# Seeding matmul banks with partial sums, and moving product 4, in a mixture kernel of seven-product quads

## The reference

```python
x = attention(q, k, v, n_global, n_local)      # banded, with 8 global keys
x = x.transpose(0, 2, 1, 3).reshape(1536, 512)
h = x @ w_in                                   # 512 -> 2048
x = (h / (1 + np.exp(-h))) @ w_out             # 2048 -> 512
P = np.exp(x @ w_gate - max)                   # 1536 x 8
for _ in range(8):
    P /= P.sum(1, keepdims=True) + 1e-09
    P /= P.sum(0, keepdims=True) + 1e-09
    P *= N / E
for e in range(8):
    out += P[:, e:e+1] * (np.maximum(x @ w1[e], 0.0) @ w2[e])   # 512 -> 1024 -> 512
```

## Time and profile before

| | us |
|---|---|
| median of 3 runs | 1489.78 (1489.61 to 1491.42) |
| profiled execution | 1489.47 |
| its span, first to last instruction | 1487.7 |
| TensorE busy | 1395.9 |
| VectorE busy | 951.6 |
| ScalarE busy | 584.2 |
| GpSimd busy | 338.2 |

### The profile page before, as it was taken

How to read it: one execution, slowest core, us unless ns; L and a number is a source line. 1 busy time by engine, 2 the same in 40 slices (tenths; PEclk the granted TensorE clock), 3 DMA queues, 4 the chain that set the end, 5 groups by cost and what they waited for, 6 DMA issues and landing times.

```text
span 1487.7 us, 20276 instructions
## 1 busy us (share of the span) xinstructions
PE 1395.9 (94%) x7339; PEld 1272.7 (86%) x7339; DVE 951.6 (64%) x1562; ACT 584.2 (39%) x1148; POOL 338.2 (23%) x377
## 2 busy tenths in 40 slices
PE   6995899999998999999999999999999999999999
PEld 5885898989997889898888989888898988889897
DVE  6455948674938584664838567783856748385662
ACT  5564727363614142332414334351433415243331
POOL 4002413130403030412214031321403123140300
PEclk9998999999989999999999999999999999999999
DMA  8310222221211121212212121231212122221201
GB/s 188 83 43 1 78 64 64 64 78 57 65 36 43 50 90 60 71 57 64 65 51 92 57 72 57 69 102 57 85 57 72 57 64 65 64 79 57 74 26 50
DMA packets 63246, 97.81 MB, mean 66 GB/s; under 512 B 18608, under 2 KB 30896, under 8 KB 63152
## 3 DMA queue, kind: packets, MB, share of 16 engines
q1 hardware_dynamic: 63152, 96.57, 21.7%
HBM read 93.41 MB, written 3.15 MB: 65 GB/s over the span
## 4 chain that ended last, share of the span: by engine, by line
PE 59%; DVE 25%; issue 3%; ACT 3%; DVEq 0%; ACTq 0%
PE a_ps L915 12%; PE c_ps L915 11%; DVE parts L1107 8%; DVE up_l L1070 8%; PE d_ps L915 6%; PE b_ps L915 6%; PE d_ps L827 5%; DVE hid_l L1114 5%; PE a_ps L827 4%; PE c_ps L827 4%; PE a_ps L912 2%; PE d_ps L912 2%; PE c_ps L912 2%; PE b_ps L827 2%; DVE down_l L1075 1%
## 5 line engine op out<-in xcount | busy, mean ns | idle before, releaser
L811 POOL TENSOR_TENSOR up_sum<-up_sum 128x256 f32<-128x256 f32 x80 | 63.1, 789 | 943.7 <-DMA up_sum<-w_up 932.0
L1075 DVE TENSOR_TENSOR down_l<-down_raw,down_h 128x512 fp32r<-128x512 f32 x160 | 112.1, 711 | 205.6 <-ACT down_h L974 205.6
L1070 DVE TENSOR_TENSOR up_l<-up_sum,up_h 128x1024 fp32r<-128x1024 f32 (+1 forms) x160 | 217.3, 1368 | 3.6 <-ACT up_h L965 3.3
L974 ACT CAST down_h<-down_raw 128x512 fp32r<-128x512 f32 x160 | 95.4, 622 | 271.4 <-PE c_ps L915 230.9
L965 ACT CAST up_h<-up_sum 128x1024 fp32r<-128x1024 f32 (+1 forms) x160 | 149.0, 943 | 40.7 <-PE d_ps L827 31.6
L827 PE MATMUL d_ps<-xc_h,up_h 128*128 128x384 f32 x320 | 112.4, 351 | 53.6 <-DVE parts L1107 53.4
L1114 DVE SCALAR_TENSOR_TENSOR hid_l<-parts,hid_h 128x384 fp32r<-128x384 f32 x192 | 144.8, 780 | 8.0
L996 ACT COPY parts<-a_ps 128x384 f32<-128x384 f32 x80 | 37.3, 466 | 256.8 <-PE a_ps L827 256.8
L1002 ACT ACTIVATE hid_h<-parts 128x384 fp32r<-128x384 f32 x192 | 94.4, 520 | 106.7 <-DVE parts L1107 106.5
L827 PE MATMUL a_ps<-xc_h,up_h 128*128 128x384 f32 x320 | 109.9, 343 | 15.9 <-DVE xc_l L1102 14.7
L827 PEld LDWEIGHTS d_ps<-xc_h,up_h 128*128 128x128 f32 x320 | 60.4, 189 | 67.6 <-DVE parts L1107 65.0
(11 more groups left out here) (187 smaller groups left out, 3441.7 us busy)
## 6 DMA issues: line engine op xcount, KB each, us to landing
up_sum<-w_up SPq DMA_DIRECT2D x80, 512.0 KB, 3.5
down_raw<-w_down SPq DMA_DIRECT2D x160, 256.0 KB, 2.6
q_sb<-qT SPq DMA_DIRECT2D x12, 256.0 KB, 3.5
k_sb<-kT SPq DMA_DIRECT2D x24, 128.0 KB, 3.6
v_sb<-v SPq DMA_DIRECT2D x24, 128.0 KB, 3.5
out<-acc SPq DMA_DIRECT2D x12, 256.0 KB, 2.1
vg_sb<-v SPq DMA_DIRECT2D x16, 4.0 KB, 1.6
nraw<-n_global SPq DMA_DIRECT2D x1, 1.0 KB, 2.5
```

What stands on the lines that cost most here:

```text
L811: nc.gpsimd.tensor_tensor(w[2], w[3], w[6], ALU.subtract).then_inc(up_summed, 1)
L974: nc.scalar.copy(down_h[:, tile % DOWN_BUFS, :], down_raw[:, tile % DOWN_RAWS, :]).then_inc(down_h_ready, 1)
L1070: nc.vector.tensor_tensor(up_l[:, quad % 2, lo:hi, :, :], up_sum[:, quad % 2, lo:hi, :, :], up_h[:, quad % 2, lo:hi, :, :].bitcast(F32), A ...
L1075: nc.vector.tensor_tensor(down_l[:, tile % DOWN_BUFS, :], down_raw[:, tile % DOWN_RAWS, :], down_h[:, tile % DOWN_BUFS, :].bitcast(F32), A ...
```

## The change

- *Seeds.* ScalarE copies P1 from a_ps into b_ps, and P6 and then P7 are added on top of it by TensorE, so that b_ps holds U2 and then U3. ScalarE copies U2 to parts and U3 into d_ps, and P4 is added on top of that. VectorE keeps two sums per quad, C12 and C22. Three fp32 matmuls (`open_banks`) write the three banks once at the start.
- *Product 4* of a quad runs after P1 and P5 of the next quad; that of the last quad after three outputs of the first down tile. P1 and P5 of the next step's first quad run among the outputs of the last down tile. The order is P1, P5, P4 of the quad before, P6, P2, P3, P7.
- *Weights.* Three quads of split up weights are held instead of two. The weights of the next step's first three quads are summed and split in the down part, those of the fourth in the third quad (in step 0 those of the second and third in the quad before). There are three pieces (3, 2 and 2 slots) instead of two. Down weights have two buffers of raw tiles and four of split ones.
- *Sums.* VectorE makes the sums of the weights, GpSimd those of the first two quads and the first sums of x, during the attention of the second batch.
- *SiLU steps.* The rounded part of a hidden result is made by VectorE (`tensor_copy`) instead of ScalarE.
- The output's accumulator is kept in x_sb.

The diff, cut to its core. Of functions that were rewritten only the new lines stand here.

```diff
--- before.py
+++ after.py
@@ -18,8 +18,9 @@
 I32 = mybir.dt.int32
 SLOTS = 7
-DOWN_RAWS = 4
-DOWN_BUFS = 3
+RAWS = 2
+UP_BUFS = 3
+DOWN_BUFS = 4
 FAR = 1.0e30
...
+                    def sum_up(quad):
+                        w = [up_slot(quad, n) for n in range(SLOTS)]
+                        pool.wait_ge(up_in[quad], 16)
+                        then(nc.gpsimd.tensor_tensor(w[4], w[3], w[2], ALU.add))
+                        nc.gpsimd.tensor_tensor(w[6], w[0], w[3], ALU.subtract)
+                        then(nc.gpsimd.tensor_tensor(w[5], w[4], w[0], ALU.subtract))
+                        then(nc.gpsimd.tensor_tensor(w[3], w[1], w[5], ALU.subtract))
...
+                    gather_gaps(0)
+                    for qb in range(2, QB):
+                        pack(0, qb)
+                    gather_gaps(1)
+                    for quad in range(RAWS):
+                        sum_up(quad)
+                    for qb in range(2, QB):
+                        pack(1, qb)
+                        if qb == 2:
+                            pool.wait_ge(x_ready, QB + 1)
+                        sum_x(qb - 2)
...
+            RECIPE = {"P1": (0, 0), "P5": (4, 1), "P6": (5, 2), "P2": (1, 3), "P3": (3, 4), "P7": (6, 5), "P4": (2, 6)}
+            X_SUM_SLOT = {0: 1, 1: 2, 2: 5, 3: 6}
+            X_RAW_SLOT = {0: (0, 0), 3: (1, 0), 4: (1, 1)}
+            PIECES = ((0, 3), (3, 5), (5, 7))
...
+                    def open_banks():
+                        for ps in (b_ps[0], b_ps[1], d_ps):
+                            mm = nc.tensor.matmul(ps[:, 0:HALF], ident[:], x_sb[:, 0, 0:HALF], start=True, stop=True)
+                        mm.then_inc(opened, 1)
...
+                    def multiply(quad, name, ps, add):
+                        w, x = RECIPE[name]
+                        s = quad // FP
+                        pe.wait_ge(up_ready, len(PIECES) * quad + PIECE_OF[w] + 1)
+                        if quad % FP == 0 and s in turns:
+                            pe.wait_ge(xc_ready, SLOTS * turns.index(s) + x + 1)
                         n = 0
                         for k in range(2):
                             for a, b in ((up_h, xc_h), (up_h, xc_l), (up_l, xc_h)):
+                                mm = nc.tensor.matmul(ps[:, 0:HALF], a[:, quad % UP_BUFS, w, k, :], b[:, x, k, :],
                                                       start=(n == 0 and not add), stop=(n == 5), skip_group_check=True)
                                 n += 1
                         mm.then_inc(product, 1)
...
+                    def p4(quad):
+                        pe.wait_ge(kept, 4 * quad + 4)
+                        multiply(quad, "P4", d_ps, True)
+                    def others(s, i, after):
+                        quad, side = s * FP + i, i % 2
+                        pe.wait_ge(kept, 4 * quad + 1)
+                        multiply(quad, "P6", b_ps[side], True)
+                        multiply(quad, "P2", a_ps[side], True)
+                        if "P2" in after:
+                            after["P2"]()
+                        pe.wait_ge(kept, 4 * quad + 2)
+                        multiply(quad, "P3", c_ps[side], True)
+                        pe.wait_ge(kept, 4 * quad + 3)
+                        multiply(quad, "P7", b_ps[side], True)
...
+                                    if t == 3:
+                                        p4(quad3)
                                     pe.wait_ge(*bank_free[t])
                                 for n, (a, b) in enumerate(((0, 0), (0, 1), (1, 0))):
                                     start, stop = j == 0 and n == 0, j == FT - 1 and n == 2
@@ -916,6 +945,10 @@
                                                               start=start, stop=stop)
                                 if j == FT - 1:
                                     mm.then_inc(down_done, 1)
+                                    if s + 1 < STEPS and t == len(banks) - 3:
+                                        p1(s + 1, 0)
+                                    if s + 1 < STEPS and t == len(banks) - 2:
+                                        p5(s + 1, 0)
                                 elif t == len(banks) - 1:
...
+                    def keep_p1(s, i):
+                        quad = s * FP + i
+                        act.wait_ge(product, made[quad, "P1"])
+                        if s == 0 and i == 0:
+                            act.wait_ge(opened, 1)
+                        if i >= 2:
+                            act.wait_ge(summed, 2 * (quad - 2) + 2)
+                        elif s > 0:
+                            act.wait_ge(acc_ready, outs_before[s - 1] + 3 * i + 3)
+                        nc.scalar.copy(b_ps[i % 2][:, 0:HALF], a_ps[i % 2][:, 0:HALF]).then_inc(kept, 1)
...
+                    def keep_u3(s, i):
+                        quad = s * FP + i
+                        act.wait_ge(product, made[quad, "P7"])
+                        if i > 0:
+                            act.wait_ge(hid_ready, 4 * (quad - 1) + 4)
+                        elif s > 0 and outs[s - 1] == 8:
+                            act.wait_ge(acc_ready, outs_before[s - 1] + 8)
+                        elif s > 0:
+                            act.wait_ge(hid_ready, 4 * (quad - 1) + 4)
+                        nc.scalar.copy(d_ps[:, 0:HALF], b_ps[i % 2][:, 0:HALF]).then_inc(kept, 1)
...
+                    def hidden(s, i, n, src, value, f, half):
+                        quad = s * FP + i
                         if blocks[s][1] >= HALVES:
+                            nc.scalar.activation(hid_h[:, f, half, :], src, ACT.Relu).then_inc(hid_h_ready, 1)
                         else:
+                            if quad > 0 and n in (0, 3):
+                                act.wait_ge(hid_ready, 4 * (quad - 1) + n + 1)
+                            if i == 0 and s in turns and n == 0:
+                                act.wait_ge(xc_ready, SLOTS * turns.index(s) + X_SUM_SLOT[2] + 1)
                             nc.scalar.activation(value, src, ACT.Silu).then_inc(silu_ready, 1)
...
                     def quad_work(s, i):
                         quad = s * FP + i
+                        start = s == 0 and i == 0
+                        keep_p1(s, i)
+                        if start:
+                            split_x(0, 4)
+                        if i > 0:
+                            hidden22(s, i - 1)
+                        keep_p5(s, i)
+                        if start:
+                            split_x(0, 5)
+                            split_x(0, 6)
+                        if i > 0:
+                            hidden21(s, i - 1)
+                        if i == 2:
+                            split_up(quad + 1, 0)
+                        elif i < 2:
+                            split_down(s * FT + 2 * i)
+                        keep_u2(s, i)
                         if s == GATE and i == 1:
                             exp_gate()
+                        hidden11(s, i)
+                        if i == 2:
+                            split_up(quad + 1, 1)
+                        elif i < 2:
+                            split_down(s * FT + 2 * i + 1)
+                        if s == 0 and i < 2:
+                            for piece in range(len(PIECES)):
+                                split_up(quad + 1, piece)
+                        hidden12(s, i)
+                        keep_u3(s, i)
+                        if i == 2:
+                            split_up(quad + 1, 2)
...
+                    def sum_up(quad):
+                        if quad >= QUADS:
+                            return
+                        w = [up_slot(quad, n) for n in range(SLOTS)]
+                        before = 4 * (quad - RAWS)
+                        dve.wait_ge(up_in[quad % RAWS], 16 * (quad // RAWS) + 16)
+                        nc.vector.tensor_tensor(w[4], w[3], w[2], ALU.add).then_inc(up_summed, 1)
+                        nc.vector.tensor_tensor(w[6], w[0], w[3], ALU.subtract).then_inc(up_summed, 1)
+                        dve.wait_ge(up_summed, before + 1)
+                        nc.vector.tensor_tensor(w[5], w[4], w[0], ALU.subtract).then_inc(up_summed, 1)
+                        dve.wait_ge(up_summed, before + 3)
+                        nc.vector.tensor_tensor(w[3], w[1], w[5], ALU.subtract).then_inc(up_summed, 1)
...
+                    def add12(s, i):
                         quad = s * FP + i
+                        dve.wait_ge(product, made[quad, "P3"])
+                        dve.wait_ge(kept, 4 * quad + 3)
+                        nc.vector.tensor_tensor(parts[:, C12, :], parts[:, U2, :], c_ps[i % 2][:, 0:HALF], ALU.add).then_inc(summed, 1)
+                    def add22(s, i):
+                        quad = s * FP + i
+                        dve.wait_ge(kept, 4 * quad + 4)
```

(53 more changed lines are left out.)

513 lines of the change are left out of this document (228 added, 285 removed).

## The result

| | before | after |
|---|---|---|
| median | 1489.69 (1488.49 to 1491.42, 4 runs) | 1444.70 (1443.57 to 1446.39, 4 runs) |
| span of the profiled execution | 1487.7 | 1441.9 |
| TensorE busy | 94% | 97% |

The ratio is 0.9698, with a 95% interval of 0.9681 to 0.9715: 45 us faster, where 53 were forecast. The time lies in the range, near its middle.

What follows compares the result with a forecast made beforehand. TensorE, busy 94%, was taken as the bound, its gaps mostly waits for VectorE. Gains of 41 (expert steps), 5 (start), 0 (attention), 0 (step 0), 4 (steps 1 to 3) and 3 (step 4) make 53: 1489.5 to 1437 us, range 1426 to 1460.

Steps and rivals of the forecast that it cites:

- The cause of the old loss: Expert steps: VectorE, stretched beside GpSimd, makes U3 late for product 4; each of 14 steps loses 3.07 us.
- The cure: In each quad: product 4's seed gets 2.08 us after P7 to arrive, VectorE loses three sums, GpSimd is idle.
- Expert steps: Steps 5 to 18: 0.15 us left of 3.07 lost per step, 14 x 2.9 = 41 us gained.
- The seeds: ScalarE's PSUM-to-PSUM copies: 0.48 us each; at 0.96, 0.8 us of each step lost again, 12 us in all.
- The start: Before the first product: it comes near 142.8 instead of 147.76, 5 us earlier (3 to 5.5).
- Step 0: First step: its 11.5 us of loss taken as unchanged (bounds -4 to +4).
- SiLU steps: Steps 1 to 3: loss 2.8 us in place of 4.1 each, 4 us gained (0 to 8).
- Step 4: Router's step: logits and their slow clock stay, VectorE's rounds are spread one later; 3 us gained (-2 to +7).
- GpSimd in the attention: Rival, second batch's attention: GpSimd's sums there hold VectorE, 1437 + 6 = 1443 us; chance 0.04.
- The cleaner case: Rival: expert steps at 61.83, SiLU steps at 63, steps 0 and 4 each 4 us better, about 1427; chance 0.13.
- VectorE would be late in the third quad: Rival: P4 and P6 wait, 1.5 us lost per expert step, 1 more per SiLU step, 1459 us; chance 0.24.

Runs made afterwards that it cites:

- the sums in the second quad: Changed kernel with the sums of the fourth quad's weights made in the second quad instead of the third, in all steps but the first: 1435.9 us, ratio 0.9637.

## Why the prediction was right, step by step

- *The cause of the old loss.* It was put on VectorE's stretching beside GpSimd, from two hidden parts in 2.10 us. The pair of runs without and with idle work on GpSimd (1437.3 and 1490.3) shows this alone, and that it was the whole 53 us. The row that the prediction set beside it for a form that is not stretched, hid_l from a_ps, never ran beside GpSimd; the sums with one input in PSUM bear the point out.
- *The cure.* I named the earlier arrival of U3, fewer sums on VectorE and the quiet GpSimd together and did not part them. The runs part only the last two from the rest: the order brings the gain, and the quiet GpSimd is bought at 6 us more than it gives. That it is U3's earlier arrival within the order is not shown. Seeds without the later P4 lose (1571.3 us), and with GpSimd's sums left on GpSimd the new order keeps them away from P4's quads.
- *Expert steps, 41 us.* The mechanism was right, the term mis-sized: 0.47 us are left per step over 61.83 instead of 0.15. 0.33 is VectorE's last split of the third quad (the wait I put at 0.1 shows as 0.22, the rest around it), as the sums in the second quad show; 0.14 stays without any sums and is mostly the new order. 14 x 0.32 = 4.5 us, most of the miss.
- *The seeds.* 463 to 472 ns for 480, and 13 us for a doubled one where 12 were worked out.
- *The start.* 6.4 us for 5: the first product came at 141.38, not 142.8. The three opening matmuls were slow as forecast, at a granted clock of 0.50, but they began at 137.93 where 138.9 was taken (1.0 us) and took 1.15 us each, not 1.3 (0.4 us). Columns as in the earlier trace rows:

```profile
137.90:141.40 3.50, 3.47 (x7) 1.88 (x7) 1.90 (x3) 3.50 (x6) 0.00 (x0) 0.50 0.02 5
141.40:144.40 3.00, 2.82 (x15) 2.23 (x13) 3.00 (x5) 2.70 (x5) 0.00 (x0) 0.96 0.00 0
```

- *Step 0, 0 us.* Right by luck of two halves: two waits of 3.0 us came, others went. The first of the two cost more than its length. Behind it the granted clock is 0.51, and ten matmuls start 0.32 us apart and not 0.17, which is 1.6 us; behind the second it is 1.00. Columns again as in the earlier trace rows:

```profile
151.80:155.20 3.40, 3.36 (x10) 3.36 (x11) 2.58 (x6) 1.05 (x3) 0.00 (x0) 0.51 0.53 157
```

- *SiLU steps, 2.9 us for 4.* Two errors met. The waits of P1, P5, P4 and P6 in the fourth quad come to 1.4 us a step, where 2.5 to 3 were worked out. And one wait was not seen: the eighth down bank is d_ps, which waits for VectorE's copy and difference of the last result, 4.6 us in four waits.
- *Step 4, 1.9 us for 3.* "Logits and their slow clock stay" was wrong by size: they took 18.0 us instead of 15.30. Without that the step would have gained 4.6 us.
- *The end, -1.3 us.* Neither the last step's 0.4 nor the 0.9 us from the last matmul to the end was in the sum. The 0.4 is mostly the gap of 0.33 that the sums in the second quad take away. Of the 0.9, 0.8 is the last output transfer: it starts 1.20 us behind the last matmul's start in both kernels and lands 2.1 us later before, 2.9 now, from x_sb. Why it takes longer was not tried.
- *Rivals.* GpSimd in the attention held nobody, so the nearness of its 1443 us to the measured time is chance. The last transposes of the attention on TensorE, changed kernel and then before:

```profile
131.35 0.66 PE L389 MATMUL x_ps<-ident,xn 128*128 128x128 f32 x4 [0.79 <-DVE xn L521]
```
```profile
132.40 0.66 PE L351 MATMUL x_ps<-ident,xn 128*128 128x128 f32 x4 [0.79 <-DVE xn L483]
```

  The cleaner case has a slip in its sum. The 7 us that it subtracts are the SiLU steps alone, and the 4 us each that it names for steps 0 and 4 are left out. By its own terms it is about 1420 us and not 1427, and the range should have begun there. That VectorE would be late in the third quad is true at a fifth of the price that the rival gave it.

## What to carry to other kernels

A stretched instruction shows as a mean above that of its quiet form, and its price is found by two runs, one without the neighbour's work and one with it on buffers of its own. Before a form is called untouched, look whether it ever ran beside the neighbour. Work that harms can be moved in time instead of to another engine: GpSimd's sums cost 53 us beside the third and fourth quads and 17 us (1439.0 against 1421.6) in the new order, where they start behind them. Whether two products of cover would have borne the old stretching is open. And in a strict queue, ask when the first consumer of moved work comes, before adding up the load.

## What the runs showed of the hardware

The stretch hits VectorE and not ScalarE: ScalarE's rounding of 768 columns, with its input in SBUF as well, stays at 840 ns before, 841 with GpSimd quiet and 840 with idle work on it, where 53 of them lie at least four fifths beside that work.

The granted clock of the logits (96 matmuls of 8 columns) falls at a point that differs between the profiled executions, of which each kernel has one. In the changed kernel, by stretches (clock third from the end):

```profile
419.00:422.00 3.00, 3.00 (x27) 3.00 (x26) 1.32 (x3) 0.90 (x2) 0.00 (x0) 0.92 0.32 87
422.00:437.00 15.00, 15.00 (x72) 15.00 (x72) 0.00 (x0) 0.00 (x0) 0.00 (x0) 0.50 0.00 1
```

and with the sums in the second quad, where it falls later:

```profile
419.40:424.80 5.40, 5.40 (x50) 5.40 (x49) 1.34 (x3) 0.90 (x2) 0.00 (x0) 0.99 0.16 49
424.80:435.10 10.30, 10.30 (x50) 10.30 (x49) 0.00 (x0) 0.00 (x0) 0.00 (x0) 0.50 0.01 2
```

At 0.50, the level of 1.2 GHz, a matmul takes 0.21 us, at 1.00 0.11. From the first start to the last end the same 96 take 15.7 us (sums in the second quad) to 19.1 us (product 4 in its own quad) over the variants of the changed kernel, so up to 3.4 us of a comparison of two of their profiled executions. What sets the point of the fall was not found.
